# Another order for the first three tiles of a fused attention and two-MLP kernel

## The reference, cut to what matters

```python
scores = scale * q @ k.T                       # B=2, H=8, S=768, D=64
keep = (pos_k < 4) | ((rel >= 0) & (rel < 128)) # four sink keys, window of 128
a = softmax(where(keep, scores, -1e9)); x = a @ v          # x: 1536 x 512
h = x @ w_in                                   # 512 -> 1024
solu = h * softmax(h)
ln = (solu - mean) / sqrt(var + 1e-6) * g_ln
x2 = ln @ w_out                                # 1024 -> 512
r = relu(x2 @ w2_in); out = (r * r) @ w2_out   # 512 -> 2048 -> 512
```

## Time and profile before

| | |
|---|---|
| median of three runs | 504.12 us (503.33 to 504.96) |
| the profiled execution's own time | 503.94 us |
| span of its trace | 502.1 us |
| PE busy | 489.4 us (97%) |
| DVE, ACT, POOL busy | 279.6, 212.7, 99.0 us |

### The profile page before, as it was taken

The page is one execution under the profiler, slowest core; times in us unless marked ns, Lnnn a source line. Parts: engine busy times, 40 slices in busy tenths (PEclk is TensorE's granted clock), DMA queues, the critical chain, the costliest instruction groups (busy, mean ns, idle before and its releaser), DMA issues.

```text
span 502.1 us, 7242 instructions
## 1 busy us (share of the span) xinstructions
PE 489.4 (97%) x2692; PEld 398.0 (79%) x2692; DVE 279.6 (56%) x501; ACT 212.7 (42%) x556; POOL 99.0 (20%) x138
## 2 busy tenths in 40 slices
PE   8989899999999999999999999999999999999997
PEld 6667778888788888878877888888888888888885
DVE  4999798777878878756696433332222232232232
ACT  4667556656666665624543322421211232221121
POOL 2555051020022112264994000000000000000000
PEclk9999999999999999999999999999999999999999
DMA  8921241241112100008000000020000002000002
GB/s 254 282 66 46 103 144 48 106 147 44 52 35 63 44 22 22 1 4 332 1 0 2 0 0 1 1 84 0 0 0 0 0 0 84 1 0 0 1 0 84
DMA packets 12069, 26.05 MB, mean 52 GB/s; under 512 B 1608, under 2 KB 1608, under 8 KB 11528
## 3 DMA queue, kind: packets, MB, share of 16 engines
q1 hardware_dynamic: 11736, 25.40, 15.6%
q10 hardware_dynamic: 304, 0.27, 0.2%
HBM read 22.52 MB, written 3.15 MB: 51 GB/s over the span
## 4 chain that ended last, share of the span: by engine, by line
PE 86%; DVE 11%; ACT 1%; POOL 1%; issue 1%; DVEq 0%; POOLq 0%; ACTq 0%
PE score_ps L1405 25%; PE h_ps L1417 12%; PE w_ps L1240 11%; PE h_ps L1202 11%; PE wt_ps L1417 6%; PE w_ps L1417 6%; PE o_ps L1172 3%; PE score_ps L1142 2%; PE wt_ps L1150 2%; PE wt_ps L1142 1%; PE h_ps L1230 1%; DVE prob L904 1%; PE o_ps L1268 1%; PE w_ps L1273 1%; PE o_ps L1189 1%; DVE w2out_lo L1059 1%
## 5 line engine op out<-in xcount | busy, mean ns | idle before, releaser
L1405 PE MATMUL score_ps<-x2T_hi,w2in_hi 128*128 (+1 forms) x192 | 74.9, 390 | 0.0
L1405 PE MATMUL score_ps<-x2T_hi,w2in_lo 128*128 (+1 forms) x192 | 74.7, 389 | 0.0
L1405 PE MATMUL score_ps<-x2T_lo,w2in_hi 128*128 (+1 forms) x192 | 74.7, 389 | 0.0
L1076 DVE TENSOR_TENSOR e<-e 128x512 f32<-128x512 f32 x24 | 18.5, 772 | 81.7 <-ACT e L772 81.7
L1076 DVE TENSOR_TENSOR sq<-relu 128x512 f32<-128x512 f32 x24 | 17.5, 728 | 80.5 <-ACT relu L772 80.5
L772 ACT ACTIVATE relu<-score_ps 128x512 f32<-128x512 f32 x24 | 14.3, 598 | 92.1 <-PE score_ps L1405 92.1
L772 ACT ACTIVATE e<-score_ps 128x512 f32<-128x512 f32 x24 | 14.4, 599 | 87.4 <-PE score_ps L1405 87.3
L1405 PEld LDWEIGHTS score_ps<-x2T_hi,w2in_hi 128*128 128x128 f32 x192 | 36.1, 188 | 7.5
L1405 PEld LDWEIGHTS score_ps<-x2T_hi,w2in_lo 128*128 128x128 f32 x192 | 36.0, 188 | 7.4
L1405 PEld LDWEIGHTS score_ps<-x2T_lo,w2in_hi 128*128 128x128 f32 x192 | 36.0, 188 | 7.4
L582 ACT ACTIVATE prob<-sm,nbias 128x132 f32<-128x132 f32 (+1 forms) x96 | 37.8, 396 | 0.5
(11 more groups left out here) (180 smaller groups left out, 1133.5 us busy)
## 6 DMA issues: line engine op xcount, KB each, us to landing
w2in<-w_in SPq DMA_DIRECT2D x4, 1024.0 KB, 4.9
w2out<-w_out SPq DMA_DIRECT2D x8, 512.0 KB, 7.4
V<-v SPq DMA_DIRECT2D x12, 256.0 KB, 2.6
k_raw<-kT SPq DMA_DIRECT2D x20, 132.0 KB, 2.8
q_raw<-qT SPq DMA_DIRECT2D x20, 128.0 KB, 2.8
w2in<-w_in SPq DMA_DIRECT2D x4, 512.0 KB, 6.5
w2in<-w_out SPq DMA_DIRECT2D x2, 1024.0 KB, 11.6
out<-u SPq DMA_DIRECT2D x6, 256.0 KB, 2.0
```

The costliest lines, as they stand in the source:

```text
L1076: nc.vector.tensor_tensor(sq[f % 2], relu[f % 2], relu[f % 2], ALU.mult).then_inc(sq_ready, 1)
L1405: done = mm(h2_ps[f % 2], ws[:, c, fs], xs[:, c, bass.ts(blk, BLK)], start=(c == 0 and i == 0), stop=(c == MC - 1 and i == 2))
```

## The change

The streams keep the same operations, apart from two `keep_warm` matmuls fewer and one more wait on POOL. What moves:

- POOL: `build_v_sink(0)` and `round_v_sink(0)` stand ahead of block 2's low part. The low part of tile 2's q (`QL`) is made ahead of `gather_sinks(1)`, and both `halves(1, ..)` behind it. `build_v_sink(1)` in t == 2 waits for tile 2's layer norm.
- ACT: `round_w_in(3)` goes between two copies of tile 1's scores, ahead of its exps. `hidden_exp(0)` goes behind `round_xT(1)`.
- DVE: `normalize_p(1, 1)` ahead of w_in's last low part; `split_v_sink(0)` and `split_k(2)` ahead of `hidden_max(0, ..)`; `split_xT(1)` ahead of tile 0's gates. In the second step `split_q(4)` and `normalize_p(3, 1)` come sooner.
- PE: `transpose_sinks(1)` ahead of `hidden_0(3, True)`; in the second step the last two scores of tile 3 ahead of `hidden(2, 16, 20)`, and `transpose_ln(1)` ahead of `hidden(2, 20, 24)`.

```diff
             # POOL
-            split_w_in(2)
             build_v_sink(0)
             round_v_sink(0)
+            split_w_in(2)
             round_k(2)
             round_q(2)
-            halves(1, 0)
-            gather_sinks(1)
-            halves(1, 1)
             nc.gpsimd.tensor_tensor(QL[0][:, :, :], q_raw[:, :, :], QH[0][:, :, :].bitcast(F32), ALU.subtract
                                     ).then_inc(q_split, 1)
+            gather_sinks(1)
+            halves(1, 0)
+            halves(1, 1)
...
                 if t == 2:
+                    pool.wait_ge(ln_ready, 2 * t + 2)
                     build_v_sink(1)
                     split_v_sink(1)
             # ACT, first_step and prologue
                 round_xT(1)
+                hidden_exp(0)
                 copy_earlier(2, 0)
...
             copy_earlier(1, 2)
+            round_w_in(3)
             copy_earlier(1, 3)
             bias(1, 0)
             for h in range(HG):
                 softmax_exp(1, h)
-            round_w_in(3)
             bias(1, 1)
...
-            hidden_exp(0)
-            copy_sinksT(1)
             act.wait_ge(g_loaded, 16)
             round_w_out(0, 1)
+            copy_sinksT(1)
             # DVE, first_step, second_step and prologue
+                split_xT(1)
                 gate(0, 0)
                 gate(0, 1)
                 stats(0, 0)
-                split_xT(1)
                 stats(0, 1)
...
                 row_max(3, 0)
+                split_q(4)
                 merge(3, 2)
...
                 normalize_p(3, 0)
                 split_k(4)
-                split_q(4)
+                normalize_p(3, 1)
                 hidden_max(2, 0)
                 hidden_max(2, 1)
                 hidden_max_all(2)
-                normalize_p(3, 1)
...
             normalize_p(1, 0)
+            normalize_p(1, 1)
             split_w_in(3)
-            normalize_p(1, 1)
+            split_v_sink(0)
+            split_k(2)
             hidden_max(0, 0)
             hidden_max(0, 1)
             hidden_max_all(0)
-            split_k(2)
-            split_v_sink(0)
             # PE, first_step, second_step and prologue
                 values(1, 0)
-                transpose_sinks(1)
-                keep_warm(2)
                 values(1, 1)
...
-                hidden(2, 16, 20)
                 score(3, 2)
                 score(3, 3)
+                hidden(2, 16, 20)
+                transpose_ln(1)
                 hidden(2, 20, 24)
-                transpose_ln(1)
                 project(1, 0, 16)
...
+            keep_warm(1)
             transpose_p(1, 0)
+            keep_warm(2)
+            transpose_p(1, 1)
+            transpose_sinks(1)
             hidden_0(3, True)
-            keep_warm(1)
-            transpose_p(1, 1)
-            keep_warm(2)
```

## The result

The changed kernel takes 505.57 us (median of 20 executions, 503.82 to 508.65) against 504.10 us for the kernel before (20 executions, 503.06 to 505.89). The ratio is 1.0034 [1.0022, 1.0046]: slower by 0.34%, about 1.5 us on the medians. The spread has grown from 2.8 to 4.8 us, and it has a pattern. Of the 20 executions 8 show a granted TensorE clock of 1.00 and have a median of 504.1; the 12 with a lower mean clock (0.986 to 0.997) have a median of 506.3. The mean does not say where in an execution the clock fell: one fall of 3 to 4 us makes it 0.996 or 0.997, so the four of these 12 at 0.993 or less fell for longer or more than once.

The account below looks back on a forecast made before the run. PE was taken to bound the steady part, with DVE's chain from 34 to 50 us second. Terms +0.4, +1.8 and -1.6 us gave +0.6, taken as +0.5: 504.6 us, range 502.2 to 506.1.

Parts of the forecast that it names:

- my own case: Whole kernel: 503.4 to 505.4 us, chance 0.53.
- the second step brings less: Rival: of the second step only the projection's 0.7 us is left, sum +1.5, 505.6 us; chance 0.15.
- slower: Whole kernel above 505.6 us, about 0.3% (1.5 us) being what a measurement can tell from no change; chance 0.21.
- The front: Up to T, the end of tile 1's last normalisation: 25.2 or 25.6 instead of 26.83 us; +0.4 in the sum.
- After T: Behind tile 1's last normalisation, POOL and DVE take turns; x is done 6.2 us later, spending the 1.2 to 1.6 won.
- The gates: Tile 0's gates behind tile 1's x: variance at 36.05 or 36.45 against 34.27 us, DVE late by 1.8 or 2.2.
- The second step: Hidden products cover PE's projection wait, normalize_hidden(2) returns to 1.00 us, PE's transposes start at 70.6: 1.6 us won.
- The clock: Rival: TensorE's clock falls back around 28 us, hidden(1)'s first twelve products cost +2.8 us, about 507; chance 0.08.
- The sum: Front +0.4, gates behind x +1.8, second step -1.6: +0.6 us, or +0.2 without the front; taken as +0.5.

Follow-up runs that it names:

- gates first: The changed kernel with tile 0's exps and gates ahead of x of tile 1, as in the kernel before: 503.56 us, ratio 0.9989.
- waits filled: The changed kernel with more keep_warm matmuls where TensorE waits in the first step: 505.08 us, ratio 1.0020.
- w_in's rounding back: The changed kernel with ACT's rounding of w_in's fourth block back behind the first four exps of tile 1: 506.73 us, ratio 1.0045.
- gates first and filled: The changed kernel with tile 0's exps and gates ahead of x again and more keep_warm matmuls in TensorE's waits: 503.12 us, ratio 0.9981.
- prologue and first step alone: The changed kernel with the second step put back as in the kernel before: 507.55 us, ratio 1.0060.
- half first: The changed kernel with halves(1, 0), the first pair of selects, ahead of gather_sinks(1) on POOL: 508.83 us, ratio 1.0084.
- the fastest one: The kernel before with the second step's edits and v_sink built ahead of block 2's low part: 502.29 us, ratio 0.9964.
- the one with all three edits: The changed kernel with tile 0's gates ahead of x, halves(1, 0) ahead of the gather, and more keep_warm matmuls: 504.62 us, ratio 1.0016.
- the kernel that has this step alone: The kernel before with only the second step's edits, POOL's wait included: 503.07 us, ratio 0.9978.
- half first and filled: The changed kernel with halves(1, 0) ahead of the gather on POOL and more keep_warm matmuls in TensorE's waits: 505.68 us, ratio 1.0033.

## Why the prediction came out as it did

The time, 505.57 us, lies in the range (502.2 to 506.1), and the sign was right. But of the 1.5 us I had forecast 0.5, and my own case, 503.4 to 505.4, is missed by a little; the range holds the time because it was drawn over the rivals too. 505.6 stood there as the price of the rival "the second step brings less", with only 0.7 us left of it. It brought 1.1 to 1.2, so that the number fits is luck. The change stands just at the point where I had put "slower": 505.57 against 505.6, and by the ratio 0.34% against 0.3%.

The traces divide into stretches that repeat to 0.1 us, with T as above and x for the start of `xT_hi`:

| stretch | as before | as changed |
|---|---|---|
| T to x, clock at 1.00 | 4.9 | 6.4 |
| T to x, clock fallen | none | 7.5 (7.2 with gates first) |
| x to the end of tile 0's variance | 2.57 (gates ahead) | 4.57 (gates behind) |
| variance to the end of the span | 467.8, 467.9 | 466.6 to 466.8 |

The 6.4 is in three kernels (waits filled; w_in's rounding back; gates first and filled), the 7.5 in two (changed kernel; prologue and first step alone). The kernels with the half first (7.1 to 8.5) and the fastest one (5.3) stand outside the first two lines, and the one with all three edits, at 3.2, outside the third. What varies most from execution to execution is T.

**The front** (forecast: T at 25.2 to 25.6, so 1.2 to 1.6 won). T is 27.11 in the profiled execution, where the load of w_in's fourth block and of `v_sink` landed late. With less waiting for loads (gates first, half first) T is 26.1 and 26.0. But the profiled executions of the changed kernel, of the filled one and of the one with gates first are 2.0, 1.7 and 0.8 us longer than the medians of their kernels. The medians and the stretches together give another size. At full clock the changed order loses 1.6 from T to x and 2.0 by the gates and wins 1.1 in the second step, a loss of 2.5 in all; the filled kernel is only 1.0 slower than before, which leaves about 1.5 us won up to T. The kernel with gates first and filled gives the same (a loss of 0.5, and yet 1.1 faster than before). This is an estimate from medians and stretches, and it bears the forecast out. My landing time of 14.1 us for `v_sink` was an estimate from one execution; in the ten profiled ones in which POOL waits for it, it begins between 13.8 and 18.9, half of them after 16.1. A second execution would have shown that such a time has no one value.

**After T** (forecast: fourth select at T + 4.95, x at T + 6.2). Right: 5.1, and x at T + 6.4 with the clock at 1.00. In the changed kernel's trace x came at T + 7.5; 1.1 of the missing 1.3 us are the value products and the sink's at the lower clock.

**The gates** (forecast: DVE late by 1.8 to 2.2). Right as a mechanism and in size. The variance came 4.6 us behind the start of `xT_hi` as forecast, against 2.6 before, and taking the gates back made the kernel 2.0 us faster, by more than the intervals. At full clock and with the 1.5 us won up to T, DVE is late by 2.1 (1.6 + 2.0 - 1.5). In the profiled execution it is 4.9, since T was late and the clock fell. That DVE doesn't catch up before `xT_lo` of tile 2 was right to 0.02 us.

**The second step** (forecast: 1.6 won). Right in kind, too large: 4.91 us late at its start and 3.79 at the scores behind it (77.17 against 73.38) is 1.1 won, the same as in the kernel that has this step alone. The projection's wait fell as forecast. u was ready about 0.5 later than I had it. The variance came 0.2 later, since two small operations of the statistics still waited their turn behind the selects (0.61 and 0.58 us instead of 0.15), and from there to u's first half it was 1.2 us where I had 0.9.

**The clock** is the term that the sum left out. I had it as a rival with 0.08 and a price of 2.8 us. I had argued that PE has waits of up to 1.11 us now as well and keeps its clock. The longest wait alone does not tell: the kernel with w_in's rounding back has waits of 0.48, 1.30 and 0.44 us in its trace, is busy for 3.78 us from 24 to 30, and stays at 1.00; the changed kernel has 1.27, 1.30 and 0.44, is busy for 2.57 us, and falls. That is one execution of each, and of the first kernel too most fall. The Trainium skill (TensorE: Matmul & The Clock Gate, "What's actually happening") has activity release the throttle, and I gave it too little weight; the runs agree with it, since with matmuls on zeros in its waits the changed kernel kept 1.00 in 11 of 11 executions, against 8 of 20.

**The sum.** I was 1.0 us low. About half of it is the second step, put at 1.6 and measured at 1.1 to 1.2. With that the sum is +1.0, and the filled kernel, always at full clock, is at +1.0. The other half is what lies between the filled and the changed kernel, the clock; their intervals overlap. How much the fall costs is open. It is 0.5 us between those medians and 1.1 in a trace where it falls in the first step. The 12 executions with a lower clock are 2.2 longer than the other 8, but those 8 are at +0.0, 1.0 us faster than the filled kernel. The fill costs nothing from T to x, which is 6.4 us with it and also without it in the kernel with w_in's rounding back. So the 8 must differ in something else, perhaps in when their loads landed; only one execution of each kernel has a trace, and that does not show it.

## What to carry to other kernels

Ask of each operation on the late engine whether it could run while that engine waits for something else: tile 0's gates fill a wait ahead of x and cost 2.0 us behind it. When POOL and DVE both read SBUF, count turns, whole instructions long, and move a POOL operation to where DVE works on PSUM or waits; the two edits of that kind are in the fastest kernel here, with 1.0 us (medians and traces) and 0.8 us (medians, within the intervals). Where one execution of a kernel has a trace, measure between marks inside it (T, x, the variance): such stretches repeat to 0.1 us where the whole moves by several. And when a change thins TensorE's work over several microseconds, look at the granted clock of many executions, not of one.

## What the runs showed of the hardware that I had not expected

The granted clock fell to 0.50 for 3 to 4 us without one long pause: in the changed kernel behind waits of 1.27, 1.30 and 0.44 us, with PE busy for 2.57 of the 6 us ahead. At that level eight value products take 1.07 us instead of 0.66. The same program does it in some executions only: 12 of 20 have a lower mean clock, which also counts falls elsewhere, such as the one from 9.0 to 12.4 us behind a wait of 1.68 us for a load (half first and filled).

A kernel can become faster while its clock falls: with gates first 10 of 11 executions show it. In its trace the fall costs 0.75 us from T to x (7.19 against 6.44 filled), by the medians 0.4, and the gates give back 2.0.
